# ScalarE's order in a gated stage: the next tile's input product is taken out of PSUM before this tile's gate is made

## The reference, cut to what matters

```python
# 1 attention with a decaying state, y[t] = q[t] @ state[t]
# 2 mixing: h = relu(x^T @ w_tok1) @ w_tok2; u = x + h^T; z = u + relu(u @ w_ch1) @ w_ch2
# 3 the gated stage
h = np.maximum(z @ w_in, 0.0)                       # (B, S, 1024)
conv_out = sum(conv_w[k] * hp[:, k:k + S, :] ...)   # 3 taps over the positions, hp is h with one zero at each end
gate = 1.0 / (1.0 + np.exp(-conv_out))
out = h * gate @ w_out                              # (B, S, 384)
```

## Time and profile before

| | |
|---|---|
| device time, median of 3 runs | 737.11 us (736.66 to 738.1) |
| the profiled execution | 736.35 us, its span 734.5 us |
| TensorE busy | 676.7 us, 92% of the span |
| VectorE busy | 402.2 us, 55% |
| ScalarE busy | 223.5 us, 30% |
| gated stage | about 519.2 us to the end |
| from the first out(0) of a batch to that of the next | 51.4 us, three times (531.96, 583.34, 634.71, 686.09) |

### The profile page before, as it was taken

The page is one execution under the profiler, slowest core; times in us unless marked ns, Lnnn a source line. Parts: engine busy times, 40 slices in busy tenths (PEclk is TensorE's granted clock), DMA queues, the critical chain, the costliest instruction groups (busy, mean ns, idle before and its releaser), DMA issues.

```text
span 734.5 us, 13281 instructions
## 1 busy us (share of the span) xinstructions
PE 676.7 (92%) x5120; PEld 652.1 (89%) x5120; DVE 402.2 (55%) x698; ACT 223.5 (30%) x418; POOL 155.7 (21%) x135
## 2 busy tenths in 40 slices
PE   2675799999999999999999999999899999999996
PEld 1564699999999999889999999999899999999996
DVE  5896154583345575225467232131676776776874
ACT  1442122332222232122323122121343443443542
POOL 2565213132211323012115113433100000000000
PEclk9955799999999999999999999999999999999999
DMA  4676111230132121051222027211102203100101
GB/s 119 215 175 159 25 29 49 66 98 2 66 98 65 45 85 36 2 153 33 66 66 77 1 94 279 80 65 43 65 1 86 109 0 129 65 1 1 65 1 64
DMA packets 51026, 52.82 MB, mean 72 GB/s; under 512 B 4272, under 2 KB 46512, under 8 KB 50960
## 3 DMA queue, kind: packets, MB, share of 16 engines
q1 hardware_dynamic: 50048, 48.78, 21.8%
q0 software_dynamic: 912, 3.16, 1.4%
HBM read 37.76 MB, written 14.16 MB: 71 GB/s over the span
## 4 chain that ended last, share of the span: by engine, by line
PE 81%; DVE 11%; issue 3%; ACT 2%; POOL 2%; DMA 1%; DVEq 0%; SPq 0%; ACTq 0%; POOLq 0%
PE bank L443 71%; PE bank L470 3%; PE bank L492 3%; DVE conv_acc L1001 2%; DVE p_sb L813 2%; PE bank L499 1%; PE bank L481 1%; DVE first L803 1%; PE bank L459 1%; PE bank L528 1%; DVE attn L839 1%; DVE inv_p L820 1%; DMA v_nat<-in_v_rows 1%; DVE g_l L985 1%; POOL k_raw L371 1%
## 5 line engine op out<-in xcount | busy, mean ns | idle before, releaser
L938 DVE SCALAR_TENSOR_TENSOR h_l<-bank,h_h 128x384 fp32r<-128x384 f32 x96 | 53.2, 556 | 167.5 <-ACT h_h L730 167.5
L730 ACT ACTIVATE h_h<-bank 128x384 fp32r<-128x384 f32 x96 | 47.2, 491 | 241.1 <-PE bank L443 241.1
L443 PE MATMUL bank<-h_h,w_ch_h 128*128 128x384 f32 x288 | 101.2, 351 | 0.6 <-DVE h_l L938 0.3
L443 PE MATMUL bank<-h_h,w_ch_l 128*128 128x384 f32 x288 | 96.7, 336 | 0.0
L443 PE MATMUL bank<-h_l,w_ch_h 128*128 128x384 f32 x288 | 96.6, 335 | 0.0
L443 PE MATMUL bank<-u_h,w_ch_l 128*128 128x384 f32 x288 | 96.5, 335 | 0.0
L443 PE MATMUL bank<-u_l,w_ch_h 128*128 128x384 f32 x288 | 96.3, 335 | 0.0
L443 PE MATMUL bank<-u_h,w_ch_h 128*128 128x384 f32 x288 | 96.3, 335 | 0.0
L371 POOL TENSOR_TENSOR k_raw<-k_raw,inv_p 128x512 f32<-128x512 f32 x24 | 30.8, 1282 | 221.7 <-DVE inv_p L820 221.7
L443 PE MATMUL bank<-w_out_h,g_h 128*128 128x384 f32 x192 | 65.5, 341 | 6.8 <-DVE g_l L985 6.8
L1001 DVE SCALAR_TENSOR_TENSOR conv_acc<-h_sb,conv_sb,conv_acc 128x768 f32<-128x768 f32 x64 | 65.8, 1029 | 2.2
(11 more groups left out here) (110 smaller groups left out, 1220.6 us busy)
## 6 DMA issues: line engine op xcount, KB each, us to landing
f_raw<-in_f_t SPq DMA_DIRECT2D x48, 96.0 KB, 2.6
k_raw<-in_k_t SPq DMA_DIRECT2D x48, 96.0 KB, 2.5
q_raw<-in_q_t SPq DMA_DIRECT2D x48, 96.0 KB, 2.5
v_nat<-in_v_rows SPq DMA_DIRECT2D x24, 192.0 KB, 2.7
stage<-in_moe_w_ch SPq DMA_DIRECT2D x6, 768.0 KB, 4.7
z_scratch_h<-stage SPq DMA_DIRECT2D x24, 192.0 KB, 1.9
z_scratch_l<-z_out SPq DMA_DIRECT2D x24, 192.0 KB, 1.9
z_h<-z_scratch_h SPq DMA_DIRECT2D x4, 1152.0 KB, 5.5
```

The source lines that it names most:

```text
L443: mm = pe.matmul(dst, stationary(a), moving(c), start=start and n == 0, stop=stop and n == len(parts_) - 1, **kw)
L730: act.activation(h2_hl[0][n % 2][:, :], mix[3 + n % 2][:, 0:HALF], ACT.Relu).then_inc(h2_hi, 1)
L938: dve.scalar_tensor_tensor(h2_hl[1][n % 2][:, :], mix[3 + n % 2][:, 0:HALF], 0.0, h2_hl[0][n % 2][:, :].bitcast(F32), ALU.max, ALU.subtrac ...
```

## The change

In ScalarE's order, h(f+1) now stands ahead of gate(f). h(0) of the first batch is taken before the loop, and h(0) of each next batch at the end of a batch. The y_out copies stay behind gate(0). `top_of_z(3, 1)`, which stood ahead of the gated stage, now stands behind h(1) of the first batch and ahead of its gate(0). No instruction is added or removed, and the other engines' orders are the same.

```diff
@@ ScalarE, mixed(b, nxt)
                 if nxt is not None:
                     settle(nxt)
-                top_of_z(b, 1)
+                    top_of_z(b, 1)
@@ ScalarE, the gated stage
+            def gated_h(b, f):
+                n = FF * b + f
+                wait(act, g_done, n - 1)
+                for half in range(2):
+                    wait(act, in_ps, 2 * n + half + 1)
+                    act.activation(h_sb[f % 2][:, 1 + half * HALF:1 + (half + 1) * HALF],
+                                   bank[3 + half][:, 0:HALF], ACT.Relu).then_inc(h_done, 1)
+
             def gated(b):
                 for f in range(FF):
-                    n = FF * b + f
-                    wait(act, g_done, n - 1)
-                    for half in range(2):
-                        wait(act, in_ps, 2 * n + half + 1)
-                        act.activation(h_sb[f % 2][:, 1 + half * HALF:1 + (half + 1) * HALF],
-                                       bank[3 + half][:, 0:HALF], ACT.Relu).then_inc(h_done, 1)
                     if f:
                         gated_hi(b, f - 1)
-                    wait(act, conv_step, 3 * n + 3)
+                    if f + 1 < FF:
+                        gated_h(b, f + 1)
+                    if f == 0 and b == 0:
+                        top_of_z(B - 1, 1)
+                    wait(act, conv_step, 3 * (FF * b + f) + 3)
                     act.activation(gate[f % 2][:, :], conv_acc[f % 2][:, :], ACT.Sigmoid).then_inc(gates, 1)
                     if f == 0 and b:
                         outputs(b - 1)
                 gated_hi(b, FF - 1)
+                if b + 1 < B:
+                    gated_h(b + 1, 0)
...
             act.wait_ge(padded, 2)
+            gated_h(0, 0)
             for b in range(B):
                 gated(b)
```

## The result

| | before | changed |
|---|---|---|
| median | 736.88 us (4 runs, 735.74 to 738.1) | 753.12 us (4 runs, 750.48 to 753.93) |
| ratio | | 1.0214, 95% interval 1.0184 to 1.0244 |
| profiled execution, span | 736.35, 734.5 us | 753.23, 751.5 us |
| TensorE waits in the gated stage, all | 8.8 us | 21.1 us |
| start of the stage to its first out(0) | 12.74 us | 14.53 us |

A forecast was written before the change was run, and what follows sets the result against it. TensorE, busy for nearly the whole gated stage, bounds the kernel; only its 8.8 us of waits count. 0 + 10.0 + 2.0 + 1.5 + 3.1 = 16.6 us on 736.35 gives 753.0, as a median 753.7; range 748.5 to 759.

The forecast's parts named there:

- part 1: Middle of a batch: the later gate still fits behind TensorE's work, cost 0 us, bounds 0 to 3.
- cover of 0.08 us: Middle of a batch: out(f) can start at T + 6.05, TensorE wants it at 6.24; 0.08 left after a 0.11 restart.
- 1.8 of cover: Middle of a batch before the change: gate(f) started 2.69 us before in(f+1) was done; this cover is used up.
- part 2: Change of batch: gate(6) and gate(0) held for h; 3.34 us each, three of them 10.0 us.
- The two waits: Change of batch: TensorE waits 1.34 us ahead of out(6), new, and 2.9 ahead of out(0) instead of 1.16.
- 0.17: Change of batch: TensorE waits 0.17 us more ahead of out(7), which can start 10.98 after in(7) ends.
- part 3: End of the last batch: out(7) starts 10.98 us after in(7) ends instead of 8.98, costing 2.0 us.
- part 4: Start of the gated stage: gate(0) 0.84 us late behind top_of_z, plus 0.63 from GpSimd's low_of_z; 1.5 us.
- part 5: TensorE's clock falls after long idles: 1.57 us a fall, two falls taken, 3.1 us, bounds 0 to 6.3.
- four new idles: TensorE idles of over 4 us at the start and 2.8 at each change of batch; two of four taken to fall.
- an idle of 2.37: TensorE, clock at 1.00 from 312 to 314 us: no fall followed, against one after the idle of 2.58 at the end.
- upper bound of 1.2: Start: most that GpSimd's low_of_z could cost VectorE's g_sb(0), one whole GpSimd instruction; 0.63 us was taken.

The follow-up runs named there:

- e1: Kernel before with h(f+1) ahead of gate(f) for f = 1 to 5 only, the rest as before; 736.81 us beside 735.77, ratio 1.0014.
- e6: Changed kernel with top_of_z(3, 1) moved behind gate(3) of the first batch; 752.75 us beside 736.07 of before, ratio 1.0234.
- e3: Changed kernel with gate(0) ahead of h(1) again in batches 1 to 3; 746.26 us beside 735.77 of before, ratio 1.0135.
- e11: Changed kernel with gate(6) ahead of h(7) again in all batches, plus 54 unused matmuls; 744.07 us beside 736.06 of before, ratio 1.0107.
- e4: Changed kernel with top_of_z(3, 1) back ahead of the gated stage, ahead of h(0); 753.68 us beside 735.77 of before, ratio 1.0256.
- e7: Kernel before with one edit, top_of_z(3, 1) behind gate(3) of the first batch; 734.93 us beside 736.07, ratio 0.9987.
- e9: Changed kernel run and profiled again without any edit, one execution; 756.19 us beside 735.76 of before.
- e8: Kernel before with top_of_z behind gate(3) and, batches 1 to 3, g_hi(0) between h(1)'s halves, g_lo(0) ahead of conv(1); 732.47 us, ratio 0.9949.
- e10: Changed kernel with gate(6) ahead of h(7) again in all batches, run a second time, one execution; 753.84 us beside 735.76 of before.
- e5: Changed kernel with 54 unused matmuls added in TensorE's idles ahead of in(2) and the last out(7); 748.55 us beside 736.07 of before, ratio 1.0191.
- e2: Changed kernel with gate(6) ahead of h(7) again in all four batches; 749.02 us beside 735.77 of before, ratio 1.0190.

## Why the prediction was right, step by step

The forecast of 753.7 met 753.12. The parts, in the order of the prediction:

- **The middle costs nothing (part 1).** Right: no wait in the middle of the changed kernel, and e1 is within 1.9 us of before. The cover of 0.08 us was right too. A g_lo on VectorE and its out on TensorE, in the changed kernel's second batch:

```profile
609.26 0.95 DVE L994 TENSOR_TENSOR g_l<-g_sb,g_h 128x768 fp32r<-128x768 f32 x1
```

```profile
610.46 0.33 PE L443 MATMUL bank<-w_out_h,g_h 128*128 128x384 f32 x1
```

  The distance is 1.20, the same for out(2) to out(5) of every batch, where 1.00 is the least; less the 0.11 of a restart it is 0.09. In the kernel before it is 2.80, which is the 1.8 of cover that the prediction names without its working. e6 shows what a cover so small is worth: next to nothing.
- **The change of batch, 3.34 each (part 2).** Measured 54.73 and 54.74 against 51.37 and 51.38, so 3.36. The two waits were worked out as 1.34 and 2.9 longer than a matmul's step; the matmuls on either side of each wait start 1.52 and 3.10 apart, which less 0.17 is 1.35 and 2.93. Ahead of out(7) it is 0.31, so 0.14 more than a step, where the prediction had 0.17. e3 and e11 take the two holds apart, 1.60 and 1.67.
- **The end, 2.0 (part 3).** Measured 42.30 - 40.29 = 2.01.
- **The start, 1.5 (part 4).** Measured 14.53 - 12.74 = 1.79. ScalarE's, VectorE's and GpSimd's timelines in the changed kernel:

```profile
527.28 1.34 ACT L710 ACTIVATE stage<-z_out 128x384 fp32r<-128x384 f32 x3
528.52 0.84 ACT L770 ACTIVATE gate<-conv_acc 128x768 f32<-128x768 f32 x1
```

```profile
529.39 1.29 DVE L988 TENSOR_TENSOR g_sb<-h_sb,gate 128x768 f32<-128x768 f32 x1 [2.26 <-ACT gate L770]
530.60 1.35 DVE L1007 TENSOR_SCALAR conv_acc<-h_sb,conv_sb 128x768 f32<-128x768 f32 x1
531.99 2.07 DVE L1010 SCALAR_TENSOR_TENSOR conv_acc<-h_sb,conv_sb,conv_acc 128x768 f32<-128x768 f32 x2
```

```profile
527.87 3.66 POOL L408 TENSOR_TENSOR z_out<-z_out,stage 128x384 fp32r<-128x384 f32 x3 [18.89 <-ACT stage L710]
```

  top_of_z pushed gate(0) back to 528.52 - 520.45 = 8.07 after the start of the stage from 526.57 - 519.22 = 7.35, by 0.72, where I had 0.84; top_of_z took 1.24 from its start to that of the gate, not 1.37. GpSimd's share was 1.07 where I had 0.63: not one but two instructions are slowed, g_sb(0) with 1.29 us instead of 0.96 and the first of conv(1)'s three with 1.35 instead of 0.62. e4 and e6 confirm the part as a whole. That GpSimd does it is shown by e7 for the kernel before, and by e6, where the lengthened instructions have moved with GpSimd's.
- **The clock, 3.1 for two falls (part 5).** The price was right (1.46 to 1.9 in the batches that had one), and the number a chance: one more than before in the changed kernel's first profile, three more in e9. 16.2 us in the medians, less 10.1, 2.0 and 1.8, leave 2.3 for it. Two of the four new idles were to have a fall, and one had. The argument that an idle of 2.37 had no fall behind it was weak: of the six profiles with an idle of 2.37 to 2.42 at that place, e3, e8, e10 and e11 fell there, at 313 to 314 us. That the sum met the median to 0.6 us is luck to this extent; the 756.19 of e9 is the same kernel.

In the pair of profiled executions the 17.0 us are 1.8 at the start, 10.1, 2.0, one fall of 1.9, and 1.2 that came ahead of the gated stage (it starts at 520.45 instead of 519.22). These are not due to the change: e5, with the same order on ScalarE, starts its stage at 519.23, and e9 at 520.77.

The rule of the Trainium skill ("SBUF — State Buffer", section "Who interferes with whom") is for a VectorE instruction with two SBUF inputs beside a GpSimd instruction that reads SBUF. g_sb(0) is such a one. The rule would have allowed up to the 1.2 of a whole GpSimd instruction and 0.33 was lost, so the trace agrees with it as a bound only. The other 0.73 were lost by an instruction that reads one tile and a column of taps, on which the rule for two inputs says nothing; that the prediction's upper bound of 1.2 for one instruction holds the 1.07 of both is chance.

What stays open: what decides whether the clock falls behind a given idle, and how many falls the executions had that were not profiled.

## What to carry to other kernels

Taking an early step sooner moves the engine's wait, it doesn't remove it: look at what stands behind the instruction that will now wait. ScalarE was idle 70% of the time, and 76 us of waits there were worth nothing, while one gate held at a change of batch cost 1.6 each time.

Work out the cover at the edges of a loop by itself. In the middle one more product stood between the held gate and its consumer; at tile 6, at tile 0 and at the end there was none. And a cover used up is a cost that shows only with the next edit (e6).

When an edit makes TensorE's idles longer, tell its effect on the idles and on the clock apart. e2 and e4 looked wrong by their times, and their traces and e11 showed that the gates did what was expected.

## What the runs showed of the hardware

- The clock of TensorE behind the same idle of 2.77 us ahead of out(0) fell in 11 of 18 cases (the six profiles with that idle, changed, e2, e4, e6, e9, e10: 0, 3, 2, 1, 2 and 3 of three). Behind the idle of 2.6 to 3.1 ahead of the last out(7) it fell in 7 of 11 profiles, and behind one of 2.7 and one of 3.0 at the start (e6, e4) it didn't. It fell in all five cases of an idle of 5.0, in four of them while the engine still idled, and in none of the idles of 1.2 to 1.7. With 1.9 to 2.0 it fell in e1 and e11 and not in before and e5.
- A fall cost 1.5 to 2.0 us where it lay between one out(0) and the next, and 1.5 at the end of before, changed, e4, e6 and e9 (8.1 us from the start of the last out(7) to the end of the span, against 6.6 without a fall). It cost 0.7 in e1, where TensorE had a wait of 0.7 behind it that took up the rest, and 3.8 at the end of e10.
- GpSimd's instructions lengthened VectorE's beside them by very unequal amounts: 0.33 (g_sb(0) of the changed kernel), 0.63 (a tap in before, in e7, and twice in e6) and 0.73 to 0.77 (the first instruction of a conv, changed and e6).
- Unused matmuls can keep the clock up: with 54 of them, 9.4 us of work at full speed, e5 had no fall in the profiled stage, and its median is 3.7 us nearer to before than that of the changed kernel. The intervals overlap, so the gain in time is not shown.
